# Storing the attention rows round by round: half of x early, the last rounds of the other half behind the last logits

## The reference

```python
# 1. a linear attention with decay: batch 4, 8 heads, 768 steps, head size 48
for t in range(S):
    cur = einsum('bhd,bhe->bhde', u * kt, vt)
    y[:, :, t] = einsum('bhd,bhde->bhe', rt, state + cur)
    state = w * state + einsum('bhd,bhe->bhde', kt, vt)
x = y.transpose(0, 2, 1, 3).reshape(3072, 384)
# 2. each token with x @ w_skip > 0 goes through its best of 8 experts
logits = xc @ w_gate;  e_idx = argmax(logits)
xc += gate * (relu(xc @ w1[e]) @ w2[e])      # 384 -> 1024 -> 384
# 3. gated layers
out = ((x @ w1m) * (x @ w2m) @ w3) @ w_out
```

## Time and profile before

| | us |
|---|---|
| median of 3 runs | 632.37 |
| lowest and highest of them | 630.25, 632.63 |
| the profiled execution | 630.16 |
| its span in the profile | 628.4 |
| PE busy (matmul) | 605.2, 96% |
| DVE busy | 293.9, 47% |
| ACT busy | 225.6, 36% |
| POOL busy | 148.4, 24% |

### The profile page before, as it was taken

How to read it: one execution, slowest core, us unless ns; L and a number is a source line. 1 busy time by engine, 2 the same in 40 slices (tenths; PEclk the granted TensorE clock), 3 DMA queues, 4 the chain that set the end, 5 groups by cost and what they waited for, 6 DMA issues and landing times. The chain is left out here.

```text
span 628.4 us, 17446 instructions
## 1 busy us (share of the span) xinstructions
PE 605.2 (96%) x7377; PEld 537.2 (85%) x7377; DVE 293.9 (47%) x456; ACT 225.6 (36%) x407; POOL 148.4 (24%) x183
## 2 busy tenths in 40 slices
PE   7799999699999999999999999999999999999997
PEld 7699998656899998999778888898888888888886
DVE  6478888177367787777121232232232214123222
ACT  2255555324456556554041232132232113123212
POOL 7467776234133333441150000000000000000000
PEclk9899999799999999999999999999999999999999
DMA  7678879875376565573230020011003001001001
GB/s 137 121 141 153 154 152 295 221 251 187 120 267 242 212 224 185 228 267 120 72 100 1 1 100 1 1 55 47 0 1 102 0 1 51 1 1 50 1 0 51
DMA packets 103545, 67.77 MB, mean 108 GB/s; under 512 B 78996, under 2 KB 97560, under 8 KB 103504
## 3 DMA queue, kind: packets, MB, share of 16 engines
q1 hardware_dynamic: 75568, 57.88, 30.3%
q10 hardware_dynamic: 26144, 4.74, 4.1%
q0 software_dynamic: 1792, 4.58, 1.9%
HBM read 55.92 MB, written 12.19 MB: 108 GB/s over the span
## 5 line engine op out<-in xcount | busy, mean ns | idle before, releaser
L1536 DVE TENSOR_TENSOR gl_g_sb<-gl_a_sb,gl_pab 128x512 f32<-128x512 f32 x48 | 33.0, 688 | 186.3 <-ACT gl_a_sb L1513 186.3
L1456 PE MATMUL gl_pab<-gl_xT_hi,wm_lo 128*128 128x512 f32 x288 | 112.9, 392 | 0.0
L1456 PE MATMUL gl_pab<-gl_xT_lo,wm_hi 128*128 128x512 f32 x288 | 112.8, 392 | 0.0
L1456 PE MATMUL gl_pab<-gl_xT_hi,wm_hi 128*128 128x512 f32 x288 | 112.1, 389 | 0.0
L1513 ACT ACTIVATE gl_a_sb<-gl_pab 128x512 f32<-128x512 f32 x48 | 28.7, 597 | 184.0 <-PE gl_pab L1456 184.0
L1456 PEld LDWEIGHTS gl_pab<-gl_xT_hi,wm_lo 128*128 128x128 f32 x288 | 54.0, 188 | 11.3
L1456 PEld LDWEIGHTS gl_pab<-gl_xT_hi,wm_hi 128*128 128x128 f32 x288 | 54.1, 188 | 10.6 <-DVE gl_xT_lo L1543 0.3
L1456 PEld LDWEIGHTS gl_pab<-gl_xT_lo,wm_hi 128*128 128x128 f32 x288 | 54.0, 188 | 10.5
L1222 PE MATMUL ex_ph<-ex_xT_hi,ew_w_hi 128*128 128x224 f32 x192 | 52.9, 275 | 0.0
L1222 PE MATMUL ex_ph<-ex_xT_hi,ew_w_lo 128*128 128x224 f32 x192 | 52.7, 274 | 0.0
L1222 PE MATMUL ex_ph<-ex_xT_lo,ew_w_hi 128*128 128x224 f32 x192 | 52.7, 274 | 0.0
(11 more groups left out here) (204 smaller groups left out, 1228.5 us busy)
## 6 DMA issues: line engine op xcount, KB each, us to landing
w_in<-in_moe_w SPq DMA_DIRECT2D x8, 1536.0 KB
ew_w_in<-in_moe_w SPq DMA_DIRECT2D x8, 1536.0 KB, 6.7
w_in<-in_moe_w SPq DMA_DIRECT2D x14, 512.0 KB, 8.8
k_in<-in_k SPq DMA_DIRECT2D x48, 96.0 KB
v_in<-in_v ACTq DMA_DIRECT2D x48, 96.0 KB, 3.2
r_in<-in_r SPq DMA_DIRECT2D x48, 96.0 KB
w_in<-xbuf SPq DMA_DIRECT2D x12, 384.0 KB, 4.0
out<-gl_o_sb SPq DMA_DIRECT2D x12, 384.0 KB, 2.4
```

Of the source, the lines that this page charges most:

```text
L1456: m = pe.matmul(p_ab[f % 2][w][:, :], a[:, w * KD + k, cols], b[t.slot][:, k, :], start=(k == 0 and n == 0), stop=(k == KD - 1 and n == 2))
L1536: dve.tensor_tensor(g_sb[f % 2][:, :], a_sb[f % 2][:, :], p_ab[f % 2][1][:, :], ALU.mult).then_inc(s_g, 1)
```

## The change

SP's program in `attention` has no loop any more: `schedule` is told first = NCH, so all 24 tiles are written out. A new part `store` in it, at shift -2, stores one chunk of batch pair 0 each time the tile of slot 2 has been kept: six times two DMAs of 192 KB. Behind the one for chunk 4 come fold loads 0, w_out and 1, and behind the next step's wait for 20 kept tiles, chunks 0 and 1 of batch pair 1. Chunk 5 of pair 0 follows when tile 22 is kept. Then SP waits for the copy of the last logits, issues fold load 2, and stores chunks 2 to 5 of batch pair 1. `routing` no longer stores anything, and POOL's gather waits for a new count, 32 for each of 8 chunk-pair units (256).

```diff
--- before.py
+++ after.py
@@ -101,14 +101,14 @@
         act.activation(self.wf[:, i, :], bank[:, 0:self.DM], ACT.Copy).then_inc(self.s_Wout, 1)
 
 
-def store_x(sp, env, xbuf, c, chunks, s_stored):
-
-
-    B, S, HALF = env["batch"], env["seq"], P // 2
-    for b in range(B):
-        rows = xbuf[b * S + c * P:b * S + (c + chunks) * P, :]
-        sp.dma_start(rows.rearrange("(g s) w -> s g w", s=HALF),
-                     env["x_all"][b // 2][b % 2 * HALF:(b % 2 + 1) * HALF, 2 * c:2 * (c + chunks), :]).then_inc(s_stored, 16)
+def store_x(sp, env, xbuf, pr, c, chunks):
+
+
+    S, HALF = env["seq"], P // 2
+    for jj in range(2):
+        row = (2 * pr + jj) * S
+        sp.dma_start(xbuf[row + c * P:row + (c + chunks) * P, :].rearrange("(g s) w -> s g w", s=HALF),
+                     env["x_all"][pr][jj * HALF:(jj + 1) * HALF, 2 * c:2 * (c + chunks), :]).then_inc(env["s_stored"], 16)
 
 
 def attention(nc, env, r, k, v, w, u, xbuf):
@@ -157,7 +157,7 @@
         bonus = [sb(f"bonus{i}", [P, H]) for i in range(2)]
         v_bonus = [sb(f"v_bonus{i}", [P, H, D]) for i in range(2)]
         x_nat = [sb(f"x_nat{i}", [P, 2, W]) for i in range(2)]
-        x_all, s_stored = env["x_all"], env["s_stored"]
+        x_all = env["x_all"]
         xT = [sb(f"xT{i}", [P, 2, KC, C]) for i in range(2)]
         state = [sb(f"state{i}", [P, 2, HP, DP]) for i in range(2)]
         state_sum = [sb(f"state_sum{i}", [P, 2, HP, D]) for i in range(2)]
@@ -231,9 +231,10 @@
                         extra(c, j, f)
             for n in range(-lead, NS * first):
                 step(n // NS, n % NS)
-            with eng.Fori(first, last + 1) as c:
-                for j in range(NS):
-                    step(c, j)
+            if first <= last:
+                with eng.Fori(first, last + 1) as c:
+                    for j in range(NS):
+                        step(c, j)
             for n in range(NS * (last + 1), NT + lag):
                 step(n // NS, n % NS)
 
@@ -263,12 +264,24 @@
                     sp.dma_start(u_all[:, :, :].rearrange("p h d -> p (h d)"),
                                  u.rearrange("h d -> (h d)").unsqueeze(0).broadcast_to([P, W])).then_inc(s_u, 16)
 
-            schedule(sp, ((load_rk, 4),), 4, 0)
-            fold.load(sp, [0])
-            fold.load_w_out(sp)
-            fold.load(sp, [1, 2])
-            wait(sp, s_kept, BASE + NS * env["early"])
-            store_x(sp, env, xbuf, 0, env["early"], s_stored)
+            def store(t):
+                if t.slot != 2:
+                    return
+                wait(sp, s_kept, t.done())
+                store_x(sp, env, xbuf, 0, t.chunk(), 1)
+
+            def extra(c, j, f):
+                if f is store and at(c, j, NT - NS):
+                    fold.load(sp, [0])
+                    fold.load_w_out(sp)
+                    fold.load(sp, [1])
+                if f is store and at(c, j, NT - NS + 1):
+                    wait(sp, s_kept, BASE + NT - NS)
+                    store_x(sp, env, xbuf, 1, 0, 2)
+            schedule(sp, ((load_rk, 4), (store, -2)), 4, 2, extra, NCH, NCH - 1)
+            sp.wait_ge(s_lg, 1)
+            fold.load(sp, [2])
+            store_x(sp, env, xbuf, 1, 2, NCH - 2)
 
         @block.tensor
         def _(pe):
@@ -746,7 +759,6 @@
             @block.sync
             def _(sp):
                 fold.load(sp, [3])
-                store_x(sp, env, xbuf, env["early"], NT // 4 - env["early"], env["s_stored"])
                 fold.load(sp, [4])
                 ex.load_w1(sp, 0)
                 fold.load(sp, [5, 6])
@@ -775,7 +787,7 @@
                 pool.wait_ge(s_slot, 1)
                 slot_values(pool, 2, piece[:, 0, :], s_gval)
                 pool.wait_ge(s_table, 1)
-                pool.wait_ge(env["s_stored"], 2 * 16 * env["batch"])
+                pool.wait_ge(env["s_stored"], 32 * (NT // 4 + 2))
                 for i in range(2):
                     ex.gather(pool, xbuf, 0, i, env["slot_token"][0:ex.rows(i), i:i + 1])
                 for i in range(1, 3):
@@ -1579,8 +1591,8 @@
             "ident": ident, "s_iota": s_iota, "n_logits": E + 1,
             "w_gate": moe_w_gate, "w_skip": moe_w_skip, "wm": (moe2_w1, moe2_w2),
             "fold": Fold(nc, sb, sem, ident, s_iota, moe2_w3, moe2_w_out),
-            "s_wmlo": sem("s_wmlo"), "lg": sb("lg", [P, E + 1, N // P]), "seq": S, "batch": B,
-            "s_stored": sem("s_stored"), "early": 5,
+            "s_wmlo": sem("s_wmlo"), "lg": sb("lg", [P, E + 1, N // P]), "seq": S,
+            "s_stored": sem("s_stored"),
             "slot_token": sb("slot_token", [P, NSL], I32),
             "slot_gate": sb("slot_gate", [P, NSL]),
             "n_over": sb("n_over", [P, 1], I32),
```

## The result

The changed kernel takes 626.3 us (median of 4 runs, 625.1 to 628.0) where the kernel before takes 631.8 us (4 runs, 630.3 to 632.6): a ratio of 0.9934, interval 0.9907 to 0.9961. By the ratio that is 4.2 us less, with 2.5 to 5.9 as the bounds; the two medians lie 5.5 us apart. Forecast were 627.0 us, and faster with a chance of 0.70. The profiled execution took 628.02 us; like the one before (630.16) it isn't at its kernel's median.

A forecast was written before the change was run, and what follows sets the result against it. PE, nearly always busy, bounds the kernel; it stalls at the last logits for code behind big stores. Gap 3.77 plus 0.35, 0.88, 0.40 gives 5.4; 630.16 less 5.4 is 624.8, plus 2.2 is 627.0 us; range 624.5 to 629.2, 8-in-10 up to 631.5.

The forecast's parts named there:

- Step (3): End barrier of attention: SP's last wait, load, stores and drain end at 121.7, covered by PE's 122.4 by 0.7 us.
- Step (4): Stores in SP's loop: later loads start 2.5 us late, within 9.3 us of cover; cost 0, 4.2 us if exposed.
- C: Attention's end barrier: final stores are held, SP becomes last, only 2.5 us won, 629.9 us; chance 0.10.
- Step (6): Routing: the gather's new count is reached about 127, the gather starts at 141 after the shift; covered by 14 us.
- B: Last logits: the stall stays, as q8 may be slow for any traffic; 630.9 to 632.4, say 631.5 us; chance 0.15.
- D: SP's loop: the wait for `keep` ahead of the loads starves k_dec, so the kernel is slower, 646 us; chance 0.07.
- Step (1): Last logits: without four big stores at 106.27, PE's code block comes near 116; stall 0, bounds 0 and 2 us.
- Step (2): Last logits to barrier: 3.77 us of gap, then 0.35, 0.88 and 0.40 of slower matmuls, L73 and L93; 5.4 won.
- step (5): SP's unrolled program: nobody waits for the register moves, 0; SP's own late code could cost up to 2 at the barrier.
- the 2.2 us that I carried along: Whole kernel: the median 632.37 is 2.2 above the profiled 630.16, place unknown; added to 624.8 to give 627.0.
- The sum of 5.4: Last logits to barrier: total predicted gain of 5.4 us, so PE's product ends at 122.4 instead of 127.8.

The follow-up runs named there:

- all rounds in the loop: Changed kernel with the second batch pair also stored round by round in the loop, none at 107 us or at the end; 625.3 us, ratio 0.9907.
- the later wait: Changed kernel with SP's wait in the loop set to a tile copied two turns later than the one stored; 643.1 us, ratio 1.0199.
- stores behind the barrier: Kernel before, SP's loop kept, with all stores of x moved out of the attention block to behind its barrier; 635.0 us, ratio 1.0062.
- without the store at 107: Changed kernel with the 0.79 MB store of the second batch pair moved into the last two stores; 624.4 us, ratio 0.9902.
- fillers: Changed kernel with seven more identity transposes on PE between the last tiles' logits, result unchanged; 626.6 us, ratio 0.9923.
- all-rounds pair: Changed kernel with both batch pairs stored round by round, without and with seven extra identity transposes on PE; 625.3 and 625.6 us.
- changed again: The changed kernel run and profiled once more, no edit; 626.1 us, ratio 0.9917.
- changed, third: Third profiled execution of the changed kernel, no edit; 628.4 us in one run.

## Why the prediction was right, step by step

**What held.** The place (the last logits), the cause of the gap (big stores in front of PE's code block, shown by taking them away) and the size of the whole, this last in part by luck, as the terms below show. Step (3): SP was to be through at 121.7 and was at 122.6; load and stores took 0.35 and 1.25 us instead of 0.8 and 1.54, but SP's wait for the last logits' copy ended 1.6 us later than put down, since the gap wasn't zero and the clock was low. PE, at 126.5, covered it by more than forecast, which rules out C. Step (4): 0, since k_dec never waits for a DMA in the changed kernel nor in the run with all rounds in the loop, and does with the later wait. Step (6): the gather starts at 145.48, and 499.4 to 500.3 us behind the release in all six profiles of the two kernels show that nothing in routing was won or lost. Of the rivals, B (the stall stays) is out by three profiles, D by the absence of the wait.

**Step (1) was nearly right.** The timetable ran about 1 us late: the pair for chunk 4 was issued at 103.2, not 102.4, the 0.79 MB at 107.3, not 106.3, so the engines were full up to 116, not 114.5. The code block came in 117 to 117.5 (116 to 117 in the other two), and 0.24 to 0.74 us of gap stayed. That lies within the bounds of 0 and 2. The rule weighed on it was that of the Trainium skill, "Runtime: NRT & Kernel Launch", section "Instruction fetch mechanics", by which such a crossing is mostly hidden; the runs agree where no large store stands in the queue at that time (no gap with the stores behind the barrier, without the store at 107 and with all rounds in the loop) and disagree in the kernel before (2.99 to 3.77 us).

**Step (2) is the one that failed.** It took the low clock for a consequence of the gap and put down 0.35 + 0.88 + 0.40 = 1.63 us as won with it (18 of 24 matmuls that take 0.53 take 0.40, so the 0.35 should have been 0.41). The three profiles of each kernel, as means:

- first L73 at 115.22, then 114.54: 0.7 won ahead of it
- gap 3.39, then 0.41: 3.0 won (forecast 3.77)
- rest of the stretch 10.38, then 11.14: 0.8 lost (forecast 1.63 won)
- behind 499.93, then 499.67: 0.3 won

Together 3.2 us, and the profiled times give 3.1 (630.7 less 627.6). In the profiles the clock term came out with the wrong sign: the clock fell in the changed kernel too, in two profiles for as long as before (0.84 over 112 to 133 us), in one for half of that (0.92). Before, the long gap fell into the low clock, so that part of it cost no work; now PE works through it. L93 took 3.22 to 3.91 us before and 3.73 to 4.84 after. The gap isn't needed for the fall, since the clock falls without one (stores behind the barrier, all rounds), and a gap of 0.74 us isn't enough (fillers). What does make it fall stays open. In this place PE has had short pieces of work with waits between, 1.39 us busy of the 2 in 116 to 118. The Trainium skill, "TensorE: Matmul & The Clock Gate", section "A second HAM failure mode: psum-queue depth-cycling", tells of frequent short idle times between groups of matmuls that make the clock go down and up again; the two runs with the low clock and no gap are in line with it (0.50 and 0.55 in 120 to 122 us), the run without the store at 107, with the same waits and full clock, is not. Three profiles had full clock in this stretch: both runs with fillers and the one without the store at 107, which has none. With one profile of each, and with equal clocks over all runs with and without fillers in the all-rounds pair, it is not shown that the fillers hold the clock up.

**A term that I had left at 0.** The loop and the epilogue ahead of the first L73 gave 0.7 us in the mean, where step (5) said 0. The v load that is no longer held (1.91 to 0.66 us of issue) would account for 0.4, by the one tile step read. The unrolling works against it (1.4 us slower by itself, where 0 was forecast). The start of the first L73 varies by 1.7 us among the profiles of before, so the 0.7 is not firm.

**What stays open.** The medians differ by 5.0 us (631.1 in 17 runs, 626.1 in 6) and the three profiles of each by 3.1. The other 2 us go with the granted clock of the executions. Its mean is 0.9871 in the 17 runs of before and 0.9912 in the 6 of changed, a difference of 2.6 us of full-speed time over the span (an estimate, 0.0041 of 626 us); in the profiles there is no such difference (0.986 to 0.989 before; 0.986, 0.986 and 0.992 after). At the same clock of 0.986 the changed kernel took 628.0 and 628.4 us and the kernel before 630.0 to 632.5, with 631.3 as the median of eight, so 3.1 less, as in the profiles. Whether the runs that weren't profiled lost less clock in this stretch, as step (2) wanted, or in the first 40 us, no run shows. For the same reason the 2.2 us that I carried along from the profile of before to its median had no counterpart afterwards. The sum of 5.4 was near the 5.0 by luck in part: in the profiles the gap gave 3.0 of its 3.77 us, the clock term missed by 2.4, and the 0.7 ahead of the first L73, the 0.3 behind the release and the 2 us of the clock, none of them forecast, made up for it. And the price of rival D, 646, leaves out the 2.2 us that the other cases carry; with them it is 648.

## What to carry to other kernels

When PE stands still on "issue" with its inputs there, it may be waiting for code, as it was here: look at the instruction queue's packets, and at what large stores were issued ahead (here 12 us), and spread that traffic. Small stores (two or four of 192 KB a round) in the issuing engine's loop cost nothing that could be measured here, where the next loads kept their cover; price that cover by making the wait longer once. Before you explain a difference by a profile, compare the profile's clock with that of the other runs. And don't book a low clock as the consequence of the gap beside it: ask what PE does before the fall, and take the gap away alone first.

## What the runs showed of the hardware

- From the half microsecond with q8's packet to PE's going on it took 2.0 to 2.6 us at the last logits of both kernels: 119.5-120 and 122.08, 120.5-121 and 123.11 in before; 117-117.5 and 119.45, 116-116.5 and 118.59 in changed.
- With the DMA engines idle (stores behind the barrier) that packet came in 114.0-114.5 us, without the store at 107 in 113.0-113.5, and PE did not stand still; with four stores of 960 KB queued it came in 119.5-121 (three profiles).
- ACT's v load near 103 us took 1.91, 2.06 and 0.96 us to issue in the three profiles in which SP had issued its large fold loads ahead of it, and 0.66 in the three of the changed kernel, where these come later. Two stores of SP took 2.95 us to issue at 1152 KB each, 1.25 at 768 KB each.
- The clock falls at the end of this block with and without a gap, and how long it stays low does not follow the gap: in "stores behind barrier", with no gap and the DMA engines idle, 0.83, 0.50, 0.82 in the three windows from 118 to 124 us; in "changed again", with 0.24 us of gap, 0.81, 0.50, 0.84; in "changed, third", with the same gap, 0.76, 0.50, 0.50 and then 0.53 in 124 to 126.
